# The first tile of w3 loaded, transposed and split in two halves, with the second tile's transposes behind the first products

## The chip, the cores and the metric

The kernel runs on one core of one Trainium2 chip. What counts is the time of one execution on the device in microseconds (us), and of several executions the median.

A core has engines that work side by side and meet at semaphores: TensorE (PE; its weight loads are listed apart as PEld), VectorE (DVE), ScalarE (ACT), GpSimd (POOL) and SyncE (SP), which here only issues DMAs. Each carries out its own list of instructions in order, so an instruction that waits holds up all behind it on its engine.

## The reference

Three layers stand in a row: attention in which a query sees only keys of its own hash bucket, a gated product of four matrices, and a mixture of four experts. The change lies in the weights of the second:

```python
def _moe_ref(x, w1, w2, w3, w_out) -> np.ndarray:
    a = x @ w1
    b = x @ w2
    h = a * b @ w3
    return (h @ w_out).astype(np.float32)
```

Here x has 1536 rows of 512 numbers, w1 and w2 are 512x1024, w3 is 1024x1024, w_out is 1024x512. In the attention there are 16 heads of 768 tokens with 64 numbers each; the experts have 512x1024 and 1024x512 weights. All is float32.

## The kernel before

**What happens first.** The kernel multiplies w3 by w_out once, at the very start, and uses the product (`wp_hi`, `wp_lo`) later. This takes eight steps (`it` = 0 to 7), one for each tile of 128 rows of w3. In each step TensorE transposes the tile in eight blocks of 128x128 (`transpose_w3`, through an identity matrix) into two PSUM banks; ScalarE copies the result as its high part to `w3T_hi` (`w3T_high`); VectorE subtracts that from PSUM for the low part `w3T_lo` (`w3T_low`); and TensorE multiplies (`multiply_wp`). float32 numbers are split in a high and a low part all over the kernel, and each product is made of three matmuls (`mult3`: high by high, low and high crossed both ways). So the step's product has eight blocks (`kt` = 0 to 7) of three matmuls of 512 columns, 24 in all, summed up in one bank.

**Buffers.** Tiles use two sets of buffers by turns (`par`): `w3_raw`, `w3T_hi`, `w3T_lo`, and the banks `ps01` and `ps23`. The trace calls `w3_raw` by the name `w_raw`, and in it all four PSUM tensors are `ps`.

**w_out.** It comes in four pieces of 512 KB (`stage` 0 to 3), each with the rows for two values of `kt`. ScalarE makes the high part of each (`wout_high(j)`), then VectorE the low one (`wout_low(j)`) and adds one to `wout_split`. In step 0 TensorE waits before each `kt` until `wout_split` is `kt // 2 + 1`: piece 0 for `kt` 0 and 1, piece 1 for 2 and 3, and so on.

**What sets the order.** All orders are written out by hand.
- SyncE issues the loads one after the other: tile 0 of w3, w_out pieces 0 and 1, tile 1, pieces 2 and 3, small constants, and then q, k and v of the first two heads. From then on it reloads `w3_raw` as soon as `w3T_mm` says that a tile is transposed.
- TensorE transposes tile 0 and tile 1 and only then starts the products of step 0. From step 1 on a part of the preparation of q and k (`first_prep`) and the transposes of the next tile stand between two steps.
- ScalarE: high part of tile 0, pieces 0 and 1, high part of tile 1, pieces 2 and 3.
- VectorE: low part of tile 0, pieces 0 and 1, low part of tile 1, pieces 2 and 3, then some small constants (`constants`), and then by turns `wp_low` and the low part of the next tile.
- GpSimd waits for the first q and k and splits them (`split_q`, `split_k`), each with a cast and a subtraction.

**Afterwards.** The attention runs over 8 pairs of heads, then come the gate products (a form of Strassen's method with seven products instead of eight), the product with `wp`, and the experts. There TensorE is nearly always busy. The change doesn't touch these parts.

Of the kernel before, what the change touches and what calls it, by code (L numbers as in the profile page):

```python
# [7 lines left out]
F32 = mybir.dt.float32  # L8
F32R = mybir.dt.float32r
BF16 = mybir.dt.bfloat16  # L10
ALU = mybir.AluOpType
# [9 lines left out]
def build_program(nc, q, k, v, proj, moe_w1, moe_w2, moe_w3, moe_w_out, probs, moe2_w1, moe2_w2,  # L21
                  codes, code_scalars, sum_rec, out):
    B, H, S, DH = q.shape
    D, F = moe_w1.shape
# [45 lines left out]
    with ExitStack() as ctx:  # L70
        def sem(name):
            return ctx.enter_context(nc.semaphore(name))
# [3 lines left out]
        def place(name, shape, dt, at=None):  # L76
            words = int(np.prod(shape[1:]))
            size = (words * (2 if dt == BF16 else 4) + 31) // 32 * 32
            offset = cursor[0] if at is None else at[0]
            if at is None:  # L80
                cursor[0] += size
            else:
                at[0] += size
            return nc.alloc_sbuf_tensor_at(name, shape, dt, offset=offset)
# [6 lines left out]
        w3_raw = [place(f"w3_raw{n}", [P, F], F32, w3_at) for n in range(2)]  # L91
        w3T_hi = [place(f"w3T_hi{n}", [P, FK, P], F32R, w3_at) for n in range(2)]
        w3T_lo = [place(f"w3T_lo{n}", [P, FK, P], F32R, w3_at) for n in range(2)]
# [132 lines left out]
        ps_w3T = [ps01, ps23]  # L226
# [6 lines left out]
        w3_loaded = [sem(f"w3_loaded{n}") for n in range(2)]  # L233
# [4 lines left out]
        e_loaded = [sem(f"e_loaded{n}") for n in range(SLOTS)]  # L238
        v2_loaded = [sem(f"v2_loaded{n}") for n in range(PIECES)]
        stored = sem("stored")  # L240
        zeros_set, ident_ready = sem("zeros_set"), sem("ident_ready")
        proj_hi_ready, proj_ready, code_ready = sem("proj_hi_ready"), sem("proj_ready"), sem("code_ready")
        gate_step, pool_held = sem("gate_step"), sem("pool_held")
        piece_hi, wout_split = sem("piece_hi"), sem("wout_split")
        w3T_mm, w3T_hi_done, w3T_lo_done = sem("w3T_mm"), sem("w3T_hi_done"), sem("w3T_lo_done")
# [24 lines left out]
        w3_tiles = moe_w3.rearrange("(i p) n -> i p n", p=P)  # L270
# [14 lines left out]
        def mult3(out_ps, lhs_hi, lhs_lo, rhs_hi, rhs_lo, start, stop, onto=False):  # L285

            nc.tensor.matmul(out_ps, lhs_hi, rhs_hi, start=start, stop=False, skip_group_check=onto)  # L287
            nc.tensor.matmul(out_ps, lhs_hi, rhs_lo, start=False, stop=False, skip_group_check=onto)  # L288
            return nc.tensor.matmul(out_ps, lhs_lo, rhs_hi, start=False, stop=stop, skip_group_check=onto)  # L289
# [4 lines left out]
        def _(sp):  # L294
# [77 lines left out]
                    ft = FT_ORDER[PIECES * h + p]  # L372
                    sp.dma_start(v2_raw[p][:, :], moe2_w2[e, ft * P:(ft + 1) * P, :]).then_inc(v2_loaded[p], 16)

            sp.dma_start(w3_raw[0][:, :], w3_tiles[0]).then_inc(w3_loaded[0], 16)
            for j in range(4):
                load_piece(j, tall(moe_w_out)[j])
                if j == 1:
# [285 lines left out]

        @block.scalar
        def _(act):
            def w3T_high(it, par, first):
                act.wait_ge(w3T_mm, it + 1)
                if not first:
                    act.wait_ge(wp_mm, it - 1)  # L670
                nc.scalar.copy(w3T_hi[par][:, :, :], ps_w3T[par][:, :, :]).then_inc(w3T_hi_done, 1)
# [5 lines left out]
            def wout_high(j):  # L677

                act.wait_ge(stage_loaded[j], 16)
                nc.scalar.copy(wout_hi[:, j * PIECE:(j + 1) * PIECE], stage[j][:, :]).then_inc(piece_hi, 1)  # L680
# [83 lines left out]
                    exp(1, 2)  # L764


            w3T_high(0, 0, True)
            wout_high(0)
            wout_high(1)
            w3T_high(1, 1, True)  # L770
            wout_high(2)
            wout_high(3)
# [5 lines left out]
            for it in range(1, FK):  # L778
                first_copy(2 * it - 2)
                wp_high(it - 1, (it - 1) % 2)  # L780
                first_copy(2 * it - 1)
                if it < FK - 1:
                    w3T_high(it + 1, (it + 1) % 2, False)
# [168 lines left out]
        @block.vector  # L952
        def _(dve):

            def w3T_low(it, par):
                dve.wait_ge(w3T_hi_done, it + 1)
                nc.vector.tensor_tensor(w3T_lo[par][:, :, :].rearrange("p (a c) n -> p a (c n)", a=2),
                                        ps_w3T[par][:, :, :],
                                        w3T_hi[par][:, :, :].rearrange("p (a c) n -> p a (c n)", a=2).bitcast(F32),
                                        ALU.subtract).then_inc(w3T_lo_done, 1)  # L960
# [7 lines left out]
            def wout_low(j):  # L968
                cols = slice(j * PIECE, (j + 1) * PIECE)
                dve.wait_ge(piece_hi, j + 1)  # L970
                nc.vector.tensor_tensor(wout_lo[:, cols], stage[j][:, :], wout_hi[:, cols].bitcast(F32),
                                        ALU.subtract).then_inc(wout_split, 1)
# [119 lines left out]
                    prep_code(n // GROUPS, n % GROUPS)  # L1092


            w3T_low(0, 0)
            wout_low(0)
            wout_low(1)
            w3T_low(1, 1)
            wout_low(2)
            wout_low(3)  # L1100
            constants()
            for it in range(1, FK):
                first_code(2 * it - 2)
                wp_low(it - 1, (it - 1) % 2)
                first_code(2 * it - 1)
                if it < FK - 1:
                    w3T_low(it + 1, (it + 1) % 2)
# [192 lines left out]
        def _(pe):  # L1300
# [1 line left out]


            def transpose_w3(it, par, first):
                pe.wait_ge(w3_loaded[par], 8 * it - 8 * par + 16)
                if not first:
                    pe.wait_ge(w3T_lo_done, it - 1)
                for kt in range(FK):
                    last = nc.tensor.transpose(ps_w3T[par][:, kt // 4, (kt % 4) * P:(kt % 4 + 1) * P],  # L1309
                                               w3_raw[par][:, kt * P:(kt + 1) * P], ident[:, :])  # L1310
                last.then_inc(w3T_mm, 1)

            def multiply_wp(it, par, first):
                pe.wait_ge(w3T_lo_done, it + 1)
                if not first:
                    pe.wait_ge(wp_lo_done, it - 1)
                for kt in range(FK):
                    if it == 0:
                        pe.wait_ge(wout_split, kt // 2 + 1)
                    if it == FK - 1 and kt in (2, 5):  # L1320

                        scores(kt // 3, 0, 0, kt // 3, kt == 2)
                    cols = slice(kt * D, (kt + 1) * D)
                    last = mult3(ps_wp[par], w3T_hi[par][:, kt, :], w3T_lo[par][:, kt, :],
                                 wout_hi[:, cols], wout_lo[:, cols], kt == 0, kt == FK - 1)
                last.then_inc(wp_mm, 1)
# [37 lines left out]
            def scores(g, i, s, t, first):  # L1364

                if t == 0:
                    pe.wait_ge(stacks_moved[s], 64 * (i + 1))
                if not first:
                    pe.wait_ge(score_scaled, g)
                for hf in range(2):  # L1370
                    half = slice(hf * HALF, (hf + 1) * HALF)
                    nc.tensor.matmul(ps_score[:, hf, 0:HALF], q_main[s][:, t * P:(t + 1) * P], k_main[s][:, half],  # L1372
                                     start=True, stop=False)
                    last = nc.tensor.matmul(ps_score[:, hf, 0:HALF], q_cross[s][:, t * P:(t + 1) * P],  # L1374
                                            k_cross[s][:, half], start=False, stop=True)
                last.then_inc(score_mm, 1)
# [82 lines left out]


            transpose_w3(0, 0, True)
            transpose_w3(1, 1, True)
            multiply_wp(0, 0, True)
            for it in range(1, FK):
                first_prep(2 * it - 2)
                if it < FK - 1:
                    transpose_w3(it + 1, (it + 1) % 2, False)
                first_prep(2 * it - 1)
                if it == FK - 1:
                    pe.wait_ge(w3T_lo_done, FK)  # L1470
                multiply_wp(it, it % 2, it == 1)
# [160 lines left out]
```

## Time and profile before

| what | value |
|---|---|
| median of 3 runs | 1017.78 us (1017.48 to 1018.08) |
| the profiled execution | 1016.71 us |
| its span, first to last instruction | 1014.8 us |
| TensorE busy | 991.9 us (98%) |
| VectorE busy | 638.2 us (63%) |
| ScalarE busy | 464.1 us (46%) |
| GpSimd busy | 402.9 us (40%) |
| TensorE busy in the first 30 us | 23.57 us |

The profile stems from one execution; its times are counted from the start of its span. The end of a matmul is modelled, so where matmuls follow each other closely their starts say more than their durations. The chain of waits is followed back from the last instruction and lists for each step what released it, or the instruction before it on its engine.

### The profile page before, as it was taken

What the parts mean: (1) busy time and instruction counts of PE and PEld (TensorE: products, weight loads), DVE (VectorE), ACT (ScalarE), POOL (GpSimd) and SP (SyncE); (2) the same over time, 40 slices, a digit from 0 to 9 for tenths busy, and PEclk for the clock granted to TensorE, in tenths of its full rate; (3) what the DMA queues carried; (4) which work ended last, traced back from release to release, by engine and by line L of the source; (5) the groups of instructions that cost most, each with busy time, mean ns of one, the idle gap of its engine ahead of it and who ended that gap; (6) DMA issues with size and microseconds to landing.
All of it is one profiled execution on the core that took longest, in us unless ns stands there. A gap on an engine that the chain in (4) does not pass through costs nothing.

```text
span 1014.8 us, 15947 instructions
## 1 busy us (share of the span) xinstructions
PE 991.9 (98%) x5520; PEld 922.2 (91%) x5520; DVE 638.2 (63%) x965; ACT 464.1 (46%) x871; POOL 402.9 (40%) x412
## 2 busy tenths in 40 slices
PE   7989999999998999999999999999999999999998
PEld 6879999999988999999998898989989899898997
DVE  5348889888997899198955354463544535345342
ACT  4238888878776554354543150331404215042230
POOL 4021333284533995295446051340603416034130
PEclk9999999999999999999999999999999999999999
DMA  6323333333233121010120110201102011010102
GB/s 239 94 70 95 94 102 97 113 94 93 86 87 91 52 78 43 7 57 10 34 63 21 42 42 1 63 21 43 42 1 62 21 41 41 1 61 21 41 12 112
DMA packets 56813, 60.58 MB, mean 60 GB/s; under 512 B 5600, under 2 KB 44736, under 8 KB 56768
## 3 DMA queue, kind: packets, MB, share of 16 engines
q1 hardware_dynamic: 56768, 60.00, 19.5%
q8 instruction: 26, 0.43, 0.2%
q14 instruction: 19, 0.16, 0.0%
HBM read 44.20 MB, written 3.19 MB: 47 GB/s over the span
## 4 chain that ended last, share of the span: by engine, by line
PE 89%; DVE 5%; issue 3%; ACT 2%; DMA 1%; SPq 0%; DVEq 0%; ACTq 0%
PE ps L287 23%; PE ps L288 23%; PE ps L289 23%; PE ps L1388 5%; PE ps L1401 3%; PE ps L1372 3%; PE ps L1403 3%; PE ps L1374 3%; PE ps L1345 1%; PE ps L1350 1%; DVE expo L989 1%; DVE w_lo L1023 1%; DVE hid_lo L1147 1%; ACT expo L691 1%; PE ps L1309 1%
## 5 line engine op out<-in xcount | busy, mean ns | idle before, releaser
L603 POOL TENSOR_TENSOR v_sum<-kept,kept 128x384 f32<-128x384 f32 x48 | 52.5, 1095 | 293.1 <-ACT kept L802 293.1
L1279 DVE SCALAR_TENSOR_TENSOR acc<-ps,gate,acc 128x512 f32<-128x512 f32 x96 | 72.0, 750 | 136.4 <-PE ps L289 136.4
L802 ACT COPY kept<-ps 128x384 f32<-128x384 f32 x144 | 64.1, 480 | 200.0 <-PE ps L289 199.4
L289 PE MATMUL ps<-v_hi,hid_lo 128*128 128x512 f32 x384 | 149.6, 390 | 0.0
L288 PE MATMUL ps<-v_lo,hid_hi 128*128 128x512 f32 x384 | 149.5, 389 | 0.0
L287 PE MATMUL ps<-v_hi,hid_hi 128*128 128x512 f32 x384 | 149.4, 389 | 0.0
L989 DVE TENSOR_SCALAR_CACHE_REDUCE expo<-ps 128x768 f32<-128x768 f32 x96 | 91.7, 955 | 24.7 <-PE ps L1374 24.7
L691 ACT ACTIVATE expo<-expo,neg_max 128x768 f32<-128x768 f32 x96 | 90.2, 940 | 8.3 <-DVE expo L989 6.7
L1266 DVE SCALAR_TENSOR_TENSOR hid_lo<-c,hid_hi 128x384 fp32r<-128x384 f32 x96 | 63.1, 669 | 46.2 <-ACT hid_hi L923 19.1
L1007 DVE TENSOR_TENSOR pT_lo<-ps,pT_hi 128x768 fp32r<-128x768 f32 x96 | 90.4, 947 | 1.5 <-ACT pT_hi L699 1.3
L289 PEld LDWEIGHTS ps<-v_hi,hid_lo 128*128 128x128 f32 x384 | 72.1, 188 | 15.0
L288 PEld LDWEIGHTS ps<-v_lo,hid_hi 128*128 128x128 f32 x384 | 72.1, 188 | 14.8
L287 PEld LDWEIGHTS ps<-v_hi,hid_hi 128*128 128x128 f32 x384 | 72.1, 188 | 14.8
L1128 DVE TENSOR_TENSOR u_sum<-ps,kept 128x384 f32<-128x384 f32 x48 | 26.6, 555 | 92.6 <-PE ps L289 90.7
L699 ACT CAST pT_hi<-ps 128x768 fp32r<-128x768 f32 x96 | 76.6, 799 | 14.8 <-PE ps L1388 14.4
L287 PE MATMUL ps<-xc_hi,w_hi 128*128 128x384 f32 x224 | 75.9, 339 | 1.4 <-ACT kept L802 1.4
L1388 PE MATMUL ps<-ident,expo 128*128 128x128 f32 x576 | 75.8, 273 | 0.6 <-DVE pT_lo L1007 0.6
L288 PE MATMUL ps<-xc_lo,e_hi 128*128 128x384 f32 x224 | 75.7, 338 | 0.0
L289 PE MATMUL ps<-xc_hi,e_lo 128*128 128x384 f32 x224 | 75.7, 338 | 0.0
L289 PE MATMUL ps<-xc_hi,w_lo 128*128 128x384 f32 x224 | 75.7, 338 | 0.0
L288 PE MATMUL ps<-xc_lo,w_hi 128*128 128x384 f32 x224 | 75.7, 338 | 0.0
L287 PE MATMUL ps<-xc_hi,e_hi 128*128 128x384 f32 x224 | 75.7, 338 | 0.0
(158 smaller groups left out, 2513.5 us busy)
## 6 DMA issues: line engine op xcount, KB each, us to landing
w_raw<-in_moe_w SPq DMA_DIRECT2D x64, 128.0 KB, 2.4
e_raw<-in_moe_w SPq DMA_DIRECT2D x64, 128.0 KB, 2.2
v_raw<-in_moe_w SPq DMA_DIRECT2D x32, 256.0 KB, 3.2
w_raw<-in_moe_w SPq DMA_DIRECT2D x8, 512.0 KB, 4.1
raw_q<-in_q SPq DMA_DIRECT2D x16, 192.0 KB, 2.8
raw_k<-in_k SPq DMA_DIRECT2D x16, 192.0 KB, 2.8
raw_v<-in_v SPq DMA_DIRECT2D x16, 192.0 KB, 2.7
q_main<-q_cross SPq DMA_DIRECT2D x16, 192.0 KB, 2.7
```

Of the source, the lines that this page charges most:

```text
L287: nc.tensor.matmul(out_ps, lhs_hi, rhs_hi, start=start, stop=False, skip_group_check=onto)
L288: nc.tensor.matmul(out_ps, lhs_hi, rhs_lo, start=False, stop=False, skip_group_check=onto)
L289: return nc.tensor.matmul(out_ps, lhs_lo, rhs_hi, start=False, stop=stop, skip_group_check=onto)
L603: nc.gpsimd.tensor_tensor(v_sum[:, :], kept[s][1][:, :], kept[s][2][:, :], ALU.add).then_inc(v_done, 1)
L691: nc.scalar.activation(expo[slot][:, :], expo[slot][:, :], ACT.Exp, scale=-1.0, bias=neg_max[:, slot:slot + 1], accum_out=row_sum[s][:, t: ...
L699: nc.scalar.copy(dst, ps_pT[t % 2][:, :, 0:HALF].rearrange("p a (c n) -> p a c n", n=P))\
L802: nc.scalar.copy(kept[s][n][:, :], ps[4 * s + n][:, 0:HALF]).then_inc(kept_done, 1)
L989: nc.vector.tensor_scalar(expo[slot][:, :].rearrange("p (a n) -> p a n", a=2), ps_score[:, :, 0:HALF], -SCALE, None, ALU.mult, ALU.min, ac ...
L1007: nc.vector.tensor_tensor(pT_lo[half][:, :, cols].rearrange("p (a c) n -> p a c n", a=2), ps_pT[t % 2][:, :, 0:HALF].rearrange("p a (c n) ...
L1266: nc.vector.scalar_tensor_tensor(hid_lo[:, tile, cols], src, 0.0, hid_hi[:, tile, cols].bitcast(F32), ALU.max, ALU.subtract).then_inc(hid_ ...
L1279: nc.vector.scalar_tensor_tensor(acc[:, t, :], ps[4 * ((h + t // 4) % 2) + t % 4], gate_f[:, bass.ds(t * E + e, 1)], acc[:, t, :], ALU.mul ...
L1388: last = nc.tensor.transpose(ps_pT[t % 2][:, kt // HT, (kt % HT) * P:(kt % HT + 1) * P], expo[slot][:, kt * P:(kt + 1) * P], ident[:, :])
```

## The change

Tile 0 of w3 is loaded with two DMAs, 512 columns each, the first of which has a semaphore of its own (`w3_first`). TensorE transposes blocks 0 to 3 after the first, and blocks 4 to 7 after the second. ScalarE and VectorE each handle the two halves with an instruction of their own, with semaphores for the first half (`w3T_first_mm`, `w3T_first_hi`, `w3T_first_lo`). The products of `kt` = 0 wait for the low part of the first half, and those of `kt` = 4 for that of the second. Tile 1's transposes are called in `multiply_wp(0, ...)` ahead of `kt` = 2. All later tiles are handled as before.

```diff
@@ block.sync
-            sp.dma_start(w3_raw[0][:, :], w3_tiles[0]).then_inc(w3_loaded[0], 16)
+            sp.dma_start(w3_raw[0][:, 0:F // 2], w3_tiles[0][:, 0:F // 2]).then_inc(w3_first, 16)
+            sp.dma_start(w3_raw[0][:, F // 2:F], w3_tiles[0][:, F // 2:F]).then_inc(w3_loaded[0], 16)
@@ block.scalar
+            def first_w3T_high():
+                act.wait_ge(w3T_first_mm, 1)
+                nc.scalar.copy(w3T_hi[0][:, 0:4, :].rearrange("p c n -> p (c n)"), ps_w3T[0][:, 0, :])\
+                    .then_inc(w3T_first_hi, 1)
+                act.wait_ge(w3T_mm, 1)
+                nc.scalar.copy(w3T_hi[0][:, 4:8, :].rearrange("p c n -> p (c n)"), ps_w3T[0][:, 1, :])\
+                    .then_inc(w3T_hi_done, 1)
...
-            w3T_high(0, 0, True)
+            first_w3T_high()
             wout_high(0)
             wout_high(1)
             w3T_high(1, 1, True)
@@ block.vector
+            def first_w3T_low():
+                for half, ready, done in ((0, w3T_first_hi, w3T_first_lo), (1, w3T_hi_done, w3T_lo_done)):
+                    tiles = slice(4 * half, 4 * half + 4)
+                    dve.wait_ge(ready, 1)
+                    nc.vector.tensor_tensor(w3T_lo[0][:, tiles, :].rearrange("p c n -> p (c n)"), ps_w3T[0][:, half, :],
+                                            w3T_hi[0][:, tiles, :].rearrange("p c n -> p (c n)").bitcast(F32),
+                                            ALU.subtract).then_inc(done, 1)
...
-            w3T_low(0, 0)
+            first_w3T_low()
@@ block.tensor
             def transpose_w3(it, par, first):
-                pe.wait_ge(w3_loaded[par], 8 * it - 8 * par + 16)
+                if first and it == 0:
+                    pe.wait_ge(w3_first, 16)
+                else:
+                    pe.wait_ge(w3_loaded[par], 8 * it - 8 * par + 16)
...
                 for kt in range(FK):
+                    if first and it == 0 and kt == 4:
+                        last.then_inc(w3T_first_mm, 1)
+                        pe.wait_ge(w3_loaded[par], 16)
...
             def multiply_wp(it, par, first):
-                pe.wait_ge(w3T_lo_done, it + 1)
+                if it:
+                    pe.wait_ge(w3T_lo_done, it + 1)
...
                     if it == 0:
+                        if kt == 2:
+                            transpose_w3(1, 1, True)
+                        if kt in (0, 4):
+                            pe.wait_ge(w3T_lo_done if kt else w3T_first_lo, 1)
                         pe.wait_ge(wout_split, kt // 2 + 1)
...
             transpose_w3(0, 0, True)
-            transpose_w3(1, 1, True)
             multiply_wp(0, 0, True)
```

The row of instructions on TensorE at the very start, before; `w_raw_51` and `w_raw_52` are the buffers of tile 0 and tile 1, `w3T_hi_53` and `w3T_lo_55` the two parts of tile 0:

```order
L1309 MATMUL ps<-ident,w_raw_51 128x128 [waits w3_loaded0,ident_ready]
L1309 MATMUL ps<-ident,w_raw_51 128x128 x7
L1309 MATMUL ps<-ident,w_raw_52 128x128 [waits w3_loaded1]
L1309 MATMUL ps<-ident,w_raw_52 128x128 x7
L287 MATMUL ps<-wout_hi,w3T_hi_53 128x512 [waits wout_split,w3T_lo_done]
L288 MATMUL ps<-wout_lo,w3T_hi_53 128x512
L289 MATMUL ps<-wout_hi,w3T_lo_55 128x512
L287 MATMUL ps<-wout_hi,w3T_hi_53 128x512 [waits wout_split]
L288 MATMUL ps<-wout_lo,w3T_hi_53 128x512
L289 MATMUL ps<-wout_hi,w3T_lo_55 128x512
```

and the same place after the change:

```order
L1335 MATMUL ps<-ident,w_raw_51 128x128 [waits w3_first,ident_ready]
L1335 MATMUL ps<-ident,w_raw_51 128x128 x3
L1335 MATMUL ps<-ident,w_raw_51 128x128 [waits w3_loaded0]
L1335 MATMUL ps<-ident,w_raw_51 128x128 x3
L290 MATMUL ps<-wout_hi,w3T_hi_53 128x512 [waits wout_split,w3T_first_lo]
L291 MATMUL ps<-wout_lo,w3T_hi_53 128x512
L292 MATMUL ps<-wout_hi,w3T_lo_55 128x512
L290 MATMUL ps<-wout_hi,w3T_hi_53 128x512 [waits wout_split]
L291 MATMUL ps<-wout_lo,w3T_hi_53 128x512
L292 MATMUL ps<-wout_hi,w3T_lo_55 128x512
L1335 MATMUL ps<-ident,w_raw_52 128x128 [waits w3_loaded1]
L1335 MATMUL ps<-ident,w_raw_52 128x128 x7
```

Tile 1's eight transposes have moved behind six matmuls of step 0, and tile 0's have been parted in four and four.

On ScalarE at the same place, before; `stage_72` to `stage_75` are the w_out pieces 0 to 3, and `w3T_hi_54` is tile 1's high part:

```order
L671 CAST w3T_hi_53<-ps 128x1024 [waits w3T_mm]
L680 CAST wout_hi<-stage_72 128x1024 [waits stage_loaded0]
L680 CAST wout_hi<-stage_73 128x1024 [waits stage_loaded1]
L671 CAST w3T_hi_54<-ps 128x1024 [waits w3T_mm]
L680 CAST wout_hi<-stage_74 128x1024 [waits stage_loaded2]
L680 CAST wout_hi<-stage_75 128x1024 [waits stage_loaded3]
```

and after:

```order
L673 CAST w3T_hi_53<-ps 128x512 [waits w3T_first_mm]
L676 CAST w3T_hi_53<-ps 128x512 [waits w3T_mm]
L692 CAST wout_hi<-stage_72 128x1024 [waits stage_loaded0]
L692 CAST wout_hi<-stage_73 128x1024 [waits stage_loaded1]
L683 CAST w3T_hi_54<-ps 128x1024 [waits w3T_mm]
L692 CAST wout_hi<-stage_74 128x1024 [waits stage_loaded2]
L692 CAST wout_hi<-stage_75 128x1024 [waits stage_loaded3]
```

The first cast has become two; the place of tile 1's cast between pieces 1 and 2 is the same. VectorE's list has changed in the same way.

## Rows read from the trace of the kernel before

**Rows 1.** The page, busy time of an engine with its share of the span

```profile
PE 991.9 (98%) x5520; PEld 922.2 (91%) x5520; DVE 638.2 (63%) x965; ACT 464.1 (46%) x871; POOL 402.9 (40%) x412
```

**Rows 2.** Waits of TensorE, whole span: us in total, times, longest

```profile
PE ps L1309 <- DMA w_raw<-in_moe_w: 6.4, 2, 4.2
PE ps L1372 <- DVE expo L989: 2.1, 2, 1.1
```

**Rows 3.** Timeline of TensorE: start, duration in us, instruction, count, idle before

```profile
4.23 1.94 PE L1309 MATMUL ps<-ident,w_raw 128*128 128x128 f32 x8 [4.23 <-DMA w_raw<-in_moe_w]
8.37 1.97 PE L1309 MATMUL ps<-ident,w_raw 128*128 128x128 f32 x8 [2.20 <-DMA w_raw<-in_moe_w]
9.99 0.78 PE L287 MATMUL ps<-wout_hi,w3T_hi 128*128 128x512 f32 x1
...
12.62 0.40 PE L287 MATMUL ps<-wout_hi,w3T_hi 128*128 128x512 f32 x1
...
17.09 1.04 PE L1309 MATMUL ps<-ident,w_raw 128*128 128x128 f32 x8
```

**Rows 4.** Chain of waits, 7 to 20 us: start, duration, what

```profile
2.17 6.15 DMA w_raw<-in_moe_w
...
16.70 0.23 PE ps L289
```

**Rows 5.** Windows: length, busy PE, PEld, DVE, ACT, POOL, granted clock, DMA share, GB/s

```profile
10.00:12.00 2.00, 2.00 (x7) 1.61 (x6) 1.32 (x2) 1.63 (x2) 0.00 (x0) 1.00 1.12 345
```

**Rows 6.** Timeline of ScalarE

```profile
7.11 1.05 ACT L680 CAST wout_hi<-stage 128x1024 fp32r<-128x1024 f32 x1
...
10.37 1.01 ACT L671 CAST w3T_hi<-ps 128x1024 fp32r<-128x1024 f32 x1 [1.26 <-PE ps L1309]
11.28 2.00 ACT L680 CAST wout_hi<-stage 128x1024 fp32r<-128x1024 f32 x2
...
17.67 0.60 ACT L675 CAST wp_hi<-ps 128x512 fp32r<-128x512 f32 x1
```

**Rows 7.** Timeline of VectorE

```profile
8.39 2.35 DVE L971 TENSOR_TENSOR wout_lo<-stage,wout_hi 128x1024 fp32r<-128x1024 f32 x2
...
12.56 2.66 DVE L971 TENSOR_TENSOR wout_lo<-stage,wout_hi 128x1024 fp32r<-128x1024 f32 x2
...
25.29 0.69 DVE L964 TENSOR_TENSOR wp_lo<-ps,wp_hi 128x512 fp32r<-128x512 f32 x1 [2.72 <-ACT wp_hi L675]
```

**Rows 8.** Timeline of SyncE's DMA issues: start, duration, tile, count

```profile
0.75 0.39 SPq L375 DMA_DIRECT2D w_raw<-in_moe_w  x1
1.20 0.93 SPq L297 DMA_DIRECT2D stage<-in_moe_w_out  x2
...
2.68 1.03 SPq L297 DMA_DIRECT2D stage<-in_moe_w_out  x2
```

**Rows 9.** Issue to landing, us: w3 tile 0, w_out piece 0, w_out piece 3

```profile
w_raw<-in_moe_w SPq DMA_DIRECT2D x1, 512.0 KB, 3.3
...
stage<-in_moe_w_out SPq DMA_DIRECT2D x1, 512.0 KB, 4.2
...
stage<-in_moe_w_out SPq DMA_DIRECT2D x1, 512.0 KB, 7.8
```

**Rows 10.** Timeline of TensorE's weight loads, at kt = 6

```profile
15.27 0.19 PEld L287 LDWEIGHTS ps<-wout_hi,w3T_hi 128*128 128x128 f32 x1 [0.17 <-DVE wout_lo L971]
```

**Rows 11.** The page, DMA issues: count, KB each, median us to landing

```profile
w_raw<-in_moe_w SPq DMA_DIRECT2D x64, 128.0 KB, 2.4
...
v_raw<-in_moe_w SPq DMA_DIRECT2D x32, 256.0 KB, 3.2
```

**Rows 12.** Timeline of GpSimd

```profile
12.84 1.30 POOL L471 CAST q_parts<-raw_q 128x384 fp32r<-128x384 f32 x1 [10.44 <-DMA raw_k<-in_k]
...
17.65 0.52 POOL L471 CAST q_parts<-raw_q 128x384 fp32r<-128x384 f32 x1
18.25 1.01 POOL L473 TENSOR_TENSOR q_parts<-raw_q,q_parts 128x384 fp32r<-128x384 f32 x1
```

More of the change, by code:

```diff
@@ L240, in build_program @@
         stored = sem("stored")
+        w3_first, w3T_first_mm, w3T_first_hi, w3T_first_lo = (
+            sem(n) for n in ("w3_first", "w3T_first_mm", "w3T_first_hi", "w3T_first_lo"))
         zeros_set, ident_ready = sem("zeros_set"), sem("ident_ready")
```

## The prediction

> **What bounds the kernel now.** I read the page's share of busy time first: TensorE is busy for 98% of the span [rows 1]. There is almost no room except where it waits, so a change at the start is worth what it moves TensorE's later work. The list of waits puts 6.4 us down to two waits for tiles of w3, 4.2 us until the first lands and 2.20 us ahead of the second tile's transposes [rows 2, 3].
>
> Next I read the chain of waits for 7 to 20 us [rows 4]: landing of the second w3 tile, its eight transposes, then the 24 products of tile 0, until 16.93 us. The first six take 2.63 us (9.99 to 12.62 [rows 3]), the last stand 0.23 us apart [rows 4]: the spacing falls from 0.43 or so to 0.23 us at about 12.5 us. 512 columns in 0.43 us are 1.2 GHz and in 0.23 us 2.4 GHz; the granted clock column says 1.00 in this stretch too [rows 5], so here I go by spacing. TensorE had worked without a break since 8.37 us, 4.1 us, when the clock rose.
>
> That chain hides a second one, nearly as late, and it decides this case. ScalarE and VectorE have one order each: tile 0's split, w_out pieces 0 and 1, **tile 1's split**, w_out pieces 2 and 3. In the timelines, ScalarE starts tile 1's high part at 10.37, behind the end of tile 1's transposes (8.37 + 1.97 = 10.34 [rows 3]), and then pieces 2 and 3 from 11.28 [rows 6]; VectorE finishes piece 3 at 12.56 + 2.66 = 15.22 us [rows 7]. Yet piece 3, the later, had landed at about 3.2 + 7.8 = 11.0 us [rows 8, 9]. At kt = 6 the weight loads already wait 0.17 us for piece 3 [rows 10]. So pieces 2 and 3 hang on the end of tile 1's transposes, and tile 0's products hang on pieces 2 and 3 with no slack.
>
> **The change, part by part.** All times are of the profiled execution (1016.71 us, span 1014.8; the median of the runs is 1017.78, 1.07 above).
>
> *Load in halves.* One DMA issue more; issues stand 0.45 us apart (0.75 to 1.20) [rows 8], so all behind it leaves 0.45 us later. The transfer engines are full meanwhile (share 1.12 [rows 5]), so the same bytes arrive at about the same time; I allow 0 to 0.45 us on each landing. Half a tile is 256 KB. Nearest rows: 128 KB in 2.4 us, 256 KB in 3.2 among three others of its kind [rows 11], and the whole 512 KB tile in 3.3 [rows 9]. So the first half lands 2.4 to 3.3 us after 0.75; I take 2.7, or 3.45. The second half is there with the last byte, 4.05 to 4.5; I take 4.2.
>
> *Transposes in halves.* Eight cost 1.62 us from the first to the following product (8.37 to 9.99), 0.20 each [rows 3]. First four from 3.5 to 4.3, second four to 5.15, with 0.35 us until the last result, as now (10.34 - 9.99): 5.5 instead of 6.17. Gain 0.7.
>
> *Splits in halves.* ScalarE's 128x512 cast costs 0.60 against 1.01 us for the whole tile [rows 6]; a following instruction starts some 0.1 before the end (10.37 + 1.01 against 11.28). The first half lies in the wait for the second, so piece 0 starts at 5.5 + 0.55 = 6.05 instead of 7.11. It has landed: 1.20 + 4.2 = 5.4 [rows 8, 9], at worst 5.85. Its cast takes 1.05, then VectorE's part 1.2 (two in 2.35) [rows 6, 7]: 7.15 to 8.35. VectorE's own halves (0.69 each by its 128x512 subtraction [rows 7]) end at 6.8 and are hidden. The first product starts at 8.4 instead of 9.99: **1.6 us earlier**. Piece 1 follows 1.2 later, at 9.6, before kt = 2 asks for it.
>
> *Tile 1's transposes behind the first products.* Six products now take 9.99 to 12.62, 2.63 us [rows 3]; from 8.4 they end at 11.0. Tile 1 landed at 2.17 + 6.15 = 8.32 [rows 4], so that wait is gone, and the old idle time is filled. The eight transposes then start at 11.0. All at the low clock they give their result 1.97 us later, 13.0; all at the high clock 1.04 later [rows 3], 12.05. The unbroken run again starts at 8.4, so I take the clock to rise at 12.5 as before: 12.7. That is **2.35 us later** than 10.34 (bounds 1.7 to 2.7).
>
> What is queued behind this wait: on ScalarE tile 1's high part, pieces 2 and 3, on VectorE their low parts and the constants; TensorE's kt = 4 to 7 wait for the pieces. All move by 2.35: piece 2 from 13.7 to 16.1, piece 3 from 15.2 to 17.6.
>
> *VectorE against GpSimd.* GpSimd's 384-element cast took 1.30 us beside VectorE's piece 2; later the cast took 0.52 and the subtraction behind it 1.01 [rows 12]. Two of VectorE's pieces together took 2.35, pieces 2 and 3 took 2.66, 0.3 more [rows 7]: it waited for the cast. GpSimd starts at 12.84, when its inputs land. VectorE now comes to pieces 2 and 3 only at 14.9, so GpSimd gets through q's cast and subtraction alone, and then subtractions of 1.01 us stand where a cast of 0.5 stood. Bounds: -0.3 (they never meet) to +1.2 (two meetings with a subtraction); I take +0.6, one subtraction instead of one cast. The Trainium skill (SBUF — State Buffer, section "SBUF: two separate sides") says that such a pair of instructions takes the shared port as an exclusive lock for the whole instruction. By that rule the later engine waits for the full rest of the other's instruction, which would make the term up to +0.7; the stretched cast fits it.
>
> *TensorE after that.* kt = 2 and 3 run from 12.65 to 14.0 (six at 0.23). Then a **new wait of 2.1 us** for piece 2 (16.1), six products to 17.5, and a wait for piece 3 at 17.6 + 0.6 = 18.2. Now it comes at 15.22, and what follows it is the same. Shift: 2.35 + 0.6 = 2.95, rounded to **+3.0 us**. The 1.6 us of the earlier start are spent in the new wait.
>
> *Later.* TensorE works almost without a gap from there [rows 1], and a later wait such as the one for scaled scores, 2.1 us in two [rows 2], is for VectorE work which TensorE feeds itself, so it moves along. VectorE's constants and tile 2's low part are queued behind piece 3 and move by 3.0 too; VectorE then stands idle for 2.72 us until 25.29 [rows 7], which moves likewise, so nobody waits for them. SyncE's reload of the second buffer waits for tile 1's transposes, 10.3 to 12.7; a 512 KB load takes 3.3 us alone [rows 9] and its use comes a whole tile's products later. No cost.
>
> The Trainium skill (TensorE: Matmul & The Clock Gate, "Part 4: PE-mode transpose") says that the full clock doesn't engage for transposes. The trace shows otherwise: eight took 1.94 us at 4.23 and 1.04 us at 17.09 [rows 3]. By the page they would end at 13.0 here and the sum would be +3.3.
>
> **The rivals.** *The clock is late or falls back.* The engine now stands for 2.1 us at 14.0, soon after the rise. For it: standing idle 2.2 us at 6.2, it worked at the low clock afterwards; against: it had not reached the high one before. Price: transposes 0.3 later and 12 products at 0.43 instead of 0.23 (2.4 us, some of it beside VectorE's piece 3): +3.6 to +5.5, middle 1022.3.
>
> *The clock rises earlier and GpSimd costs nothing.* If the earlier start of the products brings the rise forward to 11 us, the transposes end at 12.05 (+1.7), and without another meeting the shift is +1.4 to +2.0: 1019.5. For it: the rise now comes 2.5 us after the first product, which would be 10.9.
>
> *Not slower.* The 1.6 us gained stay, because tile 1's transposes end by 10.34 in spite of their new place, so that pieces 2 and 3 come no later. This decides at one point: a result of those transposes at 10.34 or before. It takes the high clock from about 5 us on: products 8.4 to 9.8 or some 0.3 sooner, transposes 1.04 more. Shift 0 to -0.8, 1017.4. No row shows the high clock so early.
>
> *The shift is absorbed.* TensorE's 2.1 us of waiting for the first scaled scores [rows 2] shrink to nothing, and +3.0 becomes +0.9 or less: 1018.7 down to 1017.8. Against: VectorE works there on what TensorE sends.
>
> **How the numbers follow.** Forecast (+2.2 to +3.6, at +3.0): 0.57. Clock late: 0.15. Clock early: 0.17. Absorbed: 0.07. Not slower: 0.04. Predicted: 1017.78 + 3.0 = 1020.8. The range 1019.0 to 1022.7 takes in the forecast, the early clock and most of the late clock, and leaves out about 0.18. A measurement of this kernel tells about 0.2% from no change, 2.04 us. Slower by over that: 0.57 + 0.15, or 0.72; within it: 0.17 + 0.07 and most of the last case, 0.26; faster by over that: 0.02.
>
> **What would show it.** First product near 8.4; tile 1's transposes from about 11.0 to 12.7, ScalarE's cast of it right behind; a wait of about 2 us of kt = 4 for VectorE's w_out piece; piece 3 near 18.2, tile 0's products ending near 19.9; the same distances from there to the end. I am wrong if kt = 4 doesn't wait, if spacing is 0.43 us beyond 14 us, or if the first tile's end has moved and the span has not.

## The result and the profile after

| | before | changed |
|---|---|---|
| median of 6 runs | 1017.93 us | 1022.06 us |
| lowest to highest | 1017.48 to 1019.01 | 1021.21 to 1024.66 |
| the profiled execution | 1016.71 us | 1024.66 us |
| its span | 1014.8 us | 1023.0 us |

The changed kernel is slower: ratio 1.0043, 95% interval 1.003 to 1.0056, or +4.1 us on the medians. The profiled execution is the slowest of its six, and that of before lay below all six of its own, so the 7.95 us between these two overstate the loss. They still show where it arises.

TensorE's waits over the whole span, us in total, times, longest (they answer [rows 2]):

```profile
PE ps L290 <- DVE wout_lo L991: 7.6, 2, 4.8
...
PE ps L1335 <- DMA w_raw<-in_moe_w: 3.5, 1, 3.5
PE ps L1403 <- DVE expo L1009: 2.1, 2, 1.1
```

The wait for the second tile of w3 is gone. In its place TensorE waits for VectorE's parts of w_out, 4.8 and 2.8 us. The later wait for scaled scores is exactly what it was.

The start on TensorE: start, duration, count, idle before (to set beside [rows 3]):

```profile
3.53 1.94 PE L1335 MATMUL ps<-ident,w_raw 128*128 128x128 f32 x8 [3.53 <-DMA w_raw<-in_moe_w]
...
10.28 0.77 PE L290 MATMUL ps<-wout_hi,w3T_hi 128*128 128x512 f32 x1 [4.80 <-DVE wout_lo L991]
...
12.97 1.91 PE L1335 MATMUL ps<-ident,w_raw 128*128 128x128 f32 x8
...
19.12 0.77 PE L290 MATMUL ps<-wout_hi,w3T_hi 128*128 128x512 f32 x1 [2.80 <-DVE wout_lo L991]
```

ScalarE's, VectorE's and GpSimd's timelines of the same stretch (for [rows 6, 7, 12]):

```profile
7.83 1.04 ACT L692 CAST wout_hi<-stage 128x1024 fp32r<-128x1024 f32 x1 [1.74 <-DMA stage<-in_moe_w_out]
...
14.92 1.02 ACT L683 CAST w3T_hi<-ps 128x1024 fp32r<-128x1024 f32 x1 [4.71 <-PE ps L1335]
```

```profile
17.11 3.30 DVE L991 TENSOR_TENSOR wout_lo<-stage,wout_hi 128x1024 fp32r<-128x1024 f32 x2
```

```profile
16.90 0.99 POOL L484 TENSOR_TENSOR k_parts<-raw_k,k_parts 128x384 fp32r<-128x384 f32 x1
17.84 1.50 POOL L475 CAST q_parts<-raw_q 128x384 fp32r<-128x384 f32 x1
```

Three things stand out.

1. The halves work as such: the tile's transposes start at 3.53 instead of 4.23. But ScalarE then stands 1.74 us for **w_out piece 0, which lands only at 7.8 us** (1.67 + 6.1), not at 5.4. The first product starts at 10.28, later than before.
2. Tile 1's transposes give their result at 14.90, ScalarE is right behind with 14.92, pieces 2 and 3 follow, and `kt` = 4 waits 2.80 us for piece 2. VectorE needs 3.30 us for the two pieces (1.86 and 1.52, the second starting before the first has ended), where it needed 2.66 before (1.22 and 1.52). The first runs into GpSimd's subtraction, which ends at 17.89.
3. After this wait TensorE works at half its clock. The windows show it; columns as in [rows 5]:

```profile
12.00:16.00 4.00, 4.00 (x17) 3.35 (x16) 0.03 (x1) 1.08 (x2) 1.14 (x2) 1.00 1.04 385
16.00:20.00 4.00, 1.20 (x4) 0.81 (x3) 4.00 (x3) 1.83 (x2) 3.84 (x5) 0.79 0.48 171
20.00:24.00 4.00, 4.00 (x11) 3.03 (x11) 3.93 (x12) 0.00 (x0) 3.84 (x5) 0.50 0.00 0
```

TensorE stands from 16.32 to 19.12 us, and the granted clock falls within that wait: in windows of half a microsecond it is 1.00 up to 18.0, 0.81 from 18.0 to 18.5 and 0.50 from 18.5 on. From 20 to 24 us it is 0.50, the 1.2 GHz level; in the chain of waits the last products of tile 0 stand 0.43 us apart:

```profile
23.73 0.43 PE ps L291
24.16 0.43 PE ps L292
24.58 0.64 PE ps L1376 x3
```

So tile 0 ends at 24.58 instead of 16.93. Afterwards the whole program is only moved. The wait for the one-hot codes and the first for scaled scores stand at 61.91 and 70.94 before:

```profile
61.91 0.34 PE L1354 MATMUL ps<-bits,code 128*128 128x384 bf16 x1 [0.84 <-DVE onehot L983]
...
70.94 0.44 PE L1372 MATMUL ps<-k_main,q_main 128*128 128x384 f32 x1 [1.06 <-DVE expo L989]
```

and 8.0 us later after, equally long:

```profile
69.91 0.34 PE L1385 MATMUL ps<-bits,code 128*128 128x384 bf16 x1 [0.84 <-DVE onehot L1003]
...
78.93 0.45 PE L1403 MATMUL ps<-k_main,q_main 128*128 128x384 f32 x1 [1.06 <-DVE expo L1009]
```

In this execution the steps of the loss are: the result of tile 1's transposes at 14.90 instead of 10.34, +4.56; piece 3 (17.11 + 3.30 = 20.41 instead of 15.22), +0.63 more; from there to the end of tile 0 4.17 instead of 1.71 us, +2.46, because the 12 products of `kt` = 4 to 7 stand 0.43 instead of 0.23 us apart, so that those of `kt` = 6 start only at 21.82, long after piece 3; a last 0.4 for the transposes behind, some of them at the low clock. That is the 8.0.

### The profile page after: what moved, and what is told of

Its sections match the earlier page's. It is cut to its first block, busy times and chain, and to the rows that moved or that the text cites. A ratio compares the mean times of both kernels' runs of the same rounds, so it can differ in the third digit from the quotient of the medians.

```text
span 1023.0 us, 15951 instructions
## 1 busy us (share of the span) xinstructions
PE 995.2 (97%) x5520; PEld 924.4 (90%) x5520; DVE 638.3 (62%) x966; ACT 464.4 (45%) x872; POOL 403.0 (39%) x412
## 4 chain that ended last, share of the span: by engine, by line
PE 88%; DVE 5%; issue 3%; ACT 3%; DMA 1%; DVEq 0%; SPq 0%; ACTq 0%
PE ps L290 23%; PE ps L291 23%; PE ps L292 23%; PE ps L1419 5%; PE ps L1432 3%; PE ps L1403 3%; PE ps L1434 3%; PE ps L1405 3%; PE ps L1376 1%; PE ps L1381 1%; DVE expo L1009 1%; DVE w_lo L1043 1%; DVE hid_lo L1167 1%; ACT expo L703 1%; PE ps L1335 1%
```

## The experiments

Each kernel was run beside the kernel before on the same chip; the times of before were 1017.66, 1017.75 and 1017.87 us in the three groups of four. "Clock 1.0" is the mean granted clock of a whole execution; a stretch at half clock shows as 0.996 to 0.998. Where nothing else is said, a kernel's executions lay at 0.999 or 1.0.

### The changed kernel again

No edit.

> The changed kernel once more, to see what repeats. Its profiled execution of before this run was 1024.66 us with piece 0 of w_out landing at 7.8 us (5.4 in the kernel before) and TensorE at the 1.2 GHz spacing again after a wait of 2.8 us. Theory A (the wait for w_out piece 2 behind tile 1's split is the cost, the fall of the clock comes with it): +3 to +4 us to the kernel before; executions in which the clock doesn't fall near +3, those in which it falls near +5. Theory B (the late landing of w_out is the cost, brought by the two half loads): piece 0 lands near 7.8 again.

1021.42 us, ratio 1.0038 (1.0024 to 1.0051). Piece 0 landed at 7.5 us, late again, and the clock fell again in the wait: products from 18.90 to 21.60 stand 0.43 us apart.

```profile
18.90 0.77 PE L290 MATMUL ps<-wout_hi,w3T_hi 128*128 128x512 f32 x1 [2.73 <-DVE wout_lo L991]
19.47 0.63 PE L291 MATMUL ps<-wout_lo,w3T_hi 128*128 128x512 f32 x1
...
21.60 0.49 PE L290 MATMUL ps<-wout_hi,w3T_hi 128*128 128x512 f32 x1
21.93 0.40 PE L291 MATMUL ps<-wout_lo,w3T_hi 128*128 128x512 f32 x1
```

Of the eleven executions of this kernel in both measurements, six had a clock of 0.996 to 0.998 (median 1022.99 us) and five had 1.0 (median 1021.21); one of the six, at 1021.45, lay below the slowest of the five, at 1021.83. Both theories seemed to hold in part, so they had to be parted.

### Halves alone

```diff
             transpose_w3(0, 0, True)
+            transpose_w3(1, 1, True)
             multiply_wp(0, 0, True)
...
-                        if kt == 2:
-                            transpose_w3(1, 1, True)
```

> Halves as in the change, but tile 1's transposes back ahead of the first products. Theory A: the result of tile 1's transposes is back at 10.3 to 10.8 us, w_out piece 3 at 15.2 to 15.7, and the time is the kernel before's within 0 to +0.6 us. Theory B (the two loads delay w_out by about 2 us): +1.5 to +2.5 us.

1018.9 us, ratio 1.001 (1.0001 to 1.0019): +1.2 us, between the two forecasts and barely clear of no change. Its profiled execution, the slowest of eleven, shows the loads late by 2.5 to 2.9 us: piece 0 at 8.3, tile 1 at 2.64 + 8.2, so that its transposes start at 10.88 (8.37 in [rows 3]). DMA issues, issue to landing (for [rows 9]): the two halves, piece 0, tile 1.

```profile
w_raw<-in_moe_w SPq DMA_DIRECT2D x1, 256.0 KB, 2.6
...
w_raw<-in_moe_w SPq DMA_DIRECT2D x1, 256.0 KB, 3.0
...
stage<-in_moe_w_out SPq DMA_DIRECT2D x1, 512.0 KB, 6.6
...
w_raw<-in_moe_w SPq DMA_DIRECT2D x1, 512.0 KB, 8.2
```

The halves themselves come early (3.35 and 4.2). What comes behind is late, although the issues are only 0.46 us later.

### The moved transposes alone

```diff
                     if it == 0:
+                        if kt == 2:
+                            transpose_w3(1, 1, True)
                         pe.wait_ge(wout_split, kt // 2 + 1)
...
             transpose_w3(0, 0, True)
-            transpose_w3(1, 1, True)
             multiply_wp(0, 0, True)
```

> The kernel before with the one edit that tile 1's transposes stand ahead of kt = 2; no halves. Theory A: first product at 9.65, six products to 12.3, transposes' result at 13.6 to 14.3, w_out piece 3 at 19 to 20: +3.7 to +4.5 us, and up to +6.5 where the clock falls in the wait. Theory B: w_out lands as before, so the time is within +1 us.

1021.38 us, ratio 1.0041 (1.0027 to 1.0054), +3.7 us. First product at 9.85 us, high part of tile 1 at 14.02 instead of 10.37, VectorE 3.30 us for the two pieces, and the new wait:

```profile
9.85 0.77 PE L287 MATMUL ps<-wout_hi,w3T_hi 128*128 128x512 f32 x1 [3.59 <-DVE wout_lo L971]
...
18.12 0.50 PE L287 MATMUL ps<-wout_hi,w3T_hi 128*128 128x512 f32 x1 [2.75 <-DVE wout_lo L971]
```

**Theory A holds for the greater part**: this edit alone brings a loss as large as the whole change. Here the clock stayed up in the profiled execution, after a wait of the same length as the one of 2.73 us behind which it fell; in two of five executions it fell. The three in which it stayed up have a median of 1021.13 us: without any fall of the clock, moving the transposes costs this kernel +3.5 us.

### Pieces 2 and 3 ahead of tile 1's split

```diff
             wout_high(1)
-            w3T_high(1, 1, True)
             wout_high(2)
             wout_high(3)
+            w3T_high(1, 1, True)
```

and the same on VectorE, both in the changed kernel.

> The changed kernel with ScalarE and VectorE doing w_out pieces 2 and 3 ahead of tile 1's split. Theory A: kt = 4 doesn't wait any more, tile 0's products end at 16 to 17.3 us (16.93 in the kernel before), tile 1's split is done before step 1's products ask for it at about 18.4, and the time is the kernel before's within -1.0 to +0.5 us. Theory B: the late w_out stays, +1.5 to +2.5 us.

1018.72 us, ratio 1.0009 (1.0 to 1.0018), +1.1 us, at the edge of what can be told from no change. `kt` = 4 doesn't wait. The wait for pieces 2 and 3 is what the move costs; with this order it costs nothing, in spite of the same place of the transposes. What is left is the load: piece 0 landed at 8.1 us, first product at 10.56.

### The changed kernel with one load

```diff
-            sp.dma_start(w3_raw[0][:, 0:F // 2], w3_tiles[0][:, 0:F // 2]).then_inc(w3_first, 16)
-            sp.dma_start(w3_raw[0][:, F // 2:F], w3_tiles[0][:, F // 2:F]).then_inc(w3_loaded[0], 16)
+            sp.dma_start(w3_raw[0][:, :], w3_tiles[0]).then_inc(w3_loaded[0], 16)
```

Both groups of four transposes wait for it.

> The changed kernel with tile 0 loaded by one DMA again; its transposes, splits and order stay as changed. Four kernels with the two column halves showed the transfers slow between 3.5 and 5.5 us (80 to 270 GB/s in half a microsecond, 350 to 400 in the kernels with one load) and w_out piece 0 landing at 7.5 to 8.3 us. Theory C (the two half loads slow the loads behind them): no such dip, piece 0 at 5.5, first product near 9.0, and 0.5 to 1.5 us less than the changed kernel, that is +2.3 to +3.3 us to the kernel before. Theory D (a chance of those executions): dip and time as in the changed kernel.

1020.25 us, ratio 1.0033 (1.0022 to 1.0043), +2.5 us. Piece 0 at 6.0 us, first product at 9.17. Five of its eight executions had clock 1.0, with a median of 1020.07 us, +2.3; the three others lay at 1021.76 to 1023.59. The changed kernel at clock 1.0 lay at 1021.21, so the half loads cost 1.1 us. The moved transposes alone had cost +3.5 at clock 1.0, with the same single load. This kernel differs from that one only in the halved transposes and splits: its first product starts at 9.17 instead of 9.85 us and tile 1's cast at 13.03 instead of 14.02. So the halved work does give back about 1 us. The bytes moved tell the same; transfers from 3.5 to 4.5 us, of the kernel before, of the halves alone and of this one:

```profile
DMA packets 195, 0.37 MB, mean 375 GB/s; under 512 B 14, under 2 KB 14, under 8 KB 195
```

```profile
DMA packets 61, 0.11 MB, mean 111 GB/s; under 512 B 7, under 2 KB 7, under 8 KB 61
```

```profile
DMA packets 188, 0.37 MB, mean 373 GB/s; under 512 B 7, under 2 KB 7, under 8 KB 188
```

The five profiled executions with both column halves on SyncE's queue gave 111 to 268 GB/s here and piece 0 at 6.5 to 8.3 us; every one with the single load gave 344 or more and 5.4 to 6.0. Theory C stands.

### One load and pieces first

Both edits together.

> The changed kernel with one load of tile 0 and with w_out pieces 2 and 3 split ahead of tile 1. Theory A (the whole loss lies in the pieces behind tile 1's split and in the half loads): nothing waits for either, tile 0's products end at 16.0 to 17.0 us, and the time is the kernel before's within -0.8 to +0.3 us.

1017.35 us, ratio 0.9996 (0.9987 to 1.0005). The whole loss is gone with these two. There were eleven executions, all at clock 1.0. Nothing measurable is gained over the kernel before, though the first product starts 0.8 us earlier than in [rows 3]: TensorE idles 2.97 us ahead of it, where it idled 2.20 us ahead of tile 1's transposes, and these now lie between the products. The last product of tile 0 starts at 17.38 us.

```profile
9.17 0.77 PE L290 MATMUL ps<-wout_hi,w3T_hi 128*128 128x512 f32 x1 [2.97 <-DVE wout_lo L990]
...
17.38 0.39 PE L292 MATMUL ps<-wout_hi,w3T_lo 128*128 128x512 f32 x1
```

### The wait filled

```diff
+                        if kt == 4:
+                            for n in range(9):
+                                nc.tensor.matmul(ps6[:, 0, :], w3T_hi[0][:, 0, :], wout_hi[:, 0:D],
+                                                 start=True, stop=True)
                         if kt in (0, 4):
                             pe.wait_ge(w3T_lo_done if kt else w3T_first_lo, 1)
```

> The changed kernel with nine more matmuls of 512 columns between kt = 3 and kt = 4, into a PSUM bank that nobody reads at that time; they fill 2.1 us of the wait for w_out piece 2. Theory A1 (the clock falls because the engine stands in that wait): no stretch at the 1.2 GHz spacing behind 17 us, the executions lie closer together, and the median is 0.3 to 1.2 us below the changed kernel's in spite of the added work. Theory A2 (the clock plays no part in the median): the time is the changed kernel's or up to 1 us more.

1020.96 us, ratio 1.0034 (1.0021 to 1.0048), all five executions at clock 1.0 and within 1.2 us. The median lies 0.5 us below that of the changed kernel in its repetition, and 1.1 below its first measurement. The difference of the medians alone is within the intervals; what is clear is the clock, and the next run repeats it.

### One load, the wait filled

> The changed kernel with one load of tile 0 and with nine more matmuls in the wait of kt = 4. Without the half loads and without a fall of the clock only the order of the pieces behind tile 1's split is left. In the kernel with the single load and no filling, executions with granted clock 1.0 lay at 1020.1 us and those below at 1021.8 to 1023.6. Expected: every execution at granted clock 1.0, +2.0 to +2.8 us to the kernel before. If the clock isn't caused by the wait: some executions above 1021.5 us again.

1020.39 us, ratio 1.0026 (1.0015 to 1.0037), seven executions, all at clock 1.0. With the unfilled moves (the changed kernel, its repetition, the moved transposes alone and the one load) the clock fell in 11 of 24 executions; with filled waits in 0 of 22 (this run, the last and the next). **The clock falls because TensorE stands in the new wait.** Where it falls, it costs 1.5 to 2.0 us (medians of the executions with and without a fall, in the changed kernel, the moved transposes alone and the one load). What is left with one load and the clock up is +2.3 to +2.5 us: the later pieces, less what the halved transposes and splits give back.

### GpSimd held back

```diff
                 split_q(s, 0, s, True)
+                if s == 0:
+                    pool.wait_ge(wout_split, 4)
                 split_k(s, s)
```

in the kernel of the last run.

> The kernel of the run whole_filled, in which GpSimd waits between its split of the first q and the first k until VectorE has done w_out piece 3. It prices the meeting of VectorE and GpSimd. If VectorE's two pieces (3.3 us together in the other kernels with the moved transposes, 2.35 alone) are slowed by GpSimd: 2.4 us now, piece 3 0.9 us earlier, +1.2 to +1.9 us to the kernel before. If not: pieces and time as in whole_filled.

1020.08 us, ratio 1.0022 (1.0012 to 1.0031), 0.3 us less than without (the executions of either kernel spread over 1.3 to 1.4 us). VectorE's two pieces without the hold, and with it:

```profile
15.69 3.16 DVE L990 TENSOR_TENSOR wout_lo<-stage,wout_hi 128x1024 fp32r<-128x1024 f32 x2
```

```profile
16.11 2.35 DVE L992 TENSOR_TENSOR wout_lo<-stage,wout_hi 128x1024 fp32r<-128x1024 f32 x2
```

The 0.8 us are GpSimd's doing. But only a part reaches the end: with the hold, piece 3 is there at 18.46, while the six products of `kt` = 4 and 5 keep TensorE until 18.93. Set off from the cast of tile 1's high part (13.50 and 13.92 us in the two executions), `kt` = 6 starts 5.41 us later without and 5.01 with the hold: 0.4 us. The forecast of 0.9 had taken VectorE's gain for the kernel's.

### Two row halves in the kernel before

```diff
-            sp.dma_start(w3_raw[0][:, :], w3_tiles[0]).then_inc(w3_loaded[0], 16)
+            sp.dma_start(w3_raw[0][0:P // 2, :], w3_tiles[0][0:P // 2]).then_inc(w3_first, 16)
+            sp.dma_start(w3_raw[0][P // 2:P, :], w3_tiles[0][P // 2:P]).then_inc(w3_loaded[0], 16)
```

> The kernel before with tile 0 loaded by two DMAs of 64 rows by 1024 columns; all else as before, and the transposes wait for both. One more DMA issue, but rows of 4 KB as in the single load, where the column halves have 2 KB. If the number of issues slows the loads behind: a dip between 3.5 and 5.5 us and piece 0 past 7 us, +1 us as for the halves alone. If the 2 KB rows do it: no dip, piece 0 at 5.4 to 5.9, +0 to +0.5 us.

1018.45 us, ratio 1.0008 (0.9999 to 1.0017), +0.7: between the two forecasts, and not clear of no change. Rows of 4 KB don't bring the transfers back: 223 GB/s from 3.5 to 4.5 us and piece 0 at 2.01 + 4.8 = 6.8. But these DMAs also take 0.58 us to issue instead of 0.39, the tile itself was complete only at 5.6 us, and the transfer engines were busy all the while (share 1.00, where the column halves had 0.61 to 0.81). So this run doesn't settle what slows the column halves.

### The halves in two queues

```diff
@@ block.sync
-            sp.dma_start(w3_raw[0][:, 0:F // 2], w3_tiles[0][:, 0:F // 2]).then_inc(w3_first, 16)
@@ block.scalar
+            act.dma_start(w3_raw[0][:, 0:F // 2], w3_tiles[0][:, 0:F // 2]).then_inc(w3_first, 16)
```

in the kernel with pieces first, where both on one queue had cost 1.1 us.

> The changed kernel with w_out pieces 2 and 3 ahead of tile 1's split, in which the first column half of tile 0 is loaded from ScalarE's queue and the second from SyncE's, at the same time. With both on SyncE's queue this kernel took +1.1 us and its piece 0 landed at 8.1 us. If the half loads hurt because they stand in one queue with the loads behind: piece 0 lands at 5.4 to 6.0 and the time is -0.6 to +0.3 us. If rows of 2 KB hurt wherever they are issued: piece 0 past 6.5, +0.7 to +1.3 us.

1017.51 us, ratio 1.0 (0.9991 to 1.0009). Piece 0 landed at 1.20 + 4.3 = 5.5 us. Transfers from 3.5 to 4.5 us:

```profile
DMA packets 211, 0.39 MB, mean 387 GB/s; under 512 B 22, under 2 KB 22, under 8 KB 211
```

Halves with the same 2 KB rows do no harm when one comes from another queue. **The harm comes with both half loads standing ahead of the pieces in one queue.** With two queues the pieces also leave 0.46 us earlier (1.20 instead of 1.66), but piece 0 lands 2.6 us earlier. What in the queue runs dry is open: in the halves-alone run the transfer engines were even less busy there (share 0.73 from 3.5 to 4.5 us) than in the kernel before (0.99). The early half is lost in this variant: with both at once they land at 4.35 and 4.15, as late as the whole tile.

### The order of the pieces alone, in the kernel before

> The kernel before with only w_out pieces 2 and 3 split ahead of tile 1. The wait of 0.17 us at kt = 6 goes, and tile 1's split comes at 12 to 14.6 us, ahead of its first use at 18.4. Expected: -0.4 to 0.0 us. It tells whether the 0.4 us by which the changed kernel with one load and this order lay under the kernel before need the halves and the moved transposes at all.

1017.63 us, ratio 1.0 (0.9991 to 1.0009). The wait of 0.17 us in [rows 10] was worth nothing that can be measured, and none of the three kernels without a loss is faster than the kernel before.

## Why the prediction came out as it did

**Right**: the direction, the mechanism and its place. The forecast was that pieces 2 and 3 hang on tile 1's transposes in ScalarE's and VectorE's fixed order, and that moving these costs a new wait of about 2 us at `kt` = 4. The measured waits are 2.31 to 2.80 us; the moved transposes alone bring +3.7 us, and the other order of the pieces takes the loss away. That the later waits move along held as well: they have the same lengths, 8.0 us later. The first half landed at 3.35 us (3.45 forecast). The term for VectorE against GpSimd had the right size at VectorE: 3.30 us is 0.64 more than before, +0.6 was forecast. Its reason was half right. VectorE didn't meet a subtraction instead of a cast but a subtraction and a cast: its first piece starts at 17.11, when 0.78 us of GpSimd's subtraction are left, and takes 0.64 longer than alone (1.86 against 1.22); its second takes 1.52, just as long as in the kernel before, where it also met a cast. The exclusive lock of which the Trainium skill speaks (SBUF — State Buffer, "SBUF: two separate sides") fits that.

**The size**: +3.0 was forecast, +4.1 measured, inside the range of 1019.0 to 1022.7. Two steps came out too low and one too high, so the landing in the range is in part luck.

- *"The same bytes arrive at about the same time"* is the step that failed. It allowed 0 to 0.45 us for the landings and took nothing for the time. Piece 0 came 2.4 us late in the profiled execution, the first product at 10.28 instead of 8.4, and the half loads cost 0.7 to 1.5 us in four pairs of kernels: 1.2 (halves alone against before, which also differ in the halved transposes and splits), 1.1 (changed against one load, at clock 1.0), 0.7 (the two filled kernels), 1.5 (the two with pieces first). The row that I read, a share of 1.12, lies at 10 to 12 us, and the transfers run short at 3.5 to 5.5. But reading that stretch of the trace before would not have warned me: its share from 3.5 to 4.5 us was 0.99, with 375 GB/s. The mistake was to carry a rate of the old kernel over to a queue with one more DMA at its head; there the share was 0.61.
- *The clock.* I took it to rise at 12.5 us and to stay up, and gave its fall 0.15. It fell in 6 of 11 executions of the changed kernel, at 1.8 us each, so some 1 us on the average. The rival's middle lay 1.5 us over my forecast, and 1.5 to 2.0 is what a fall costs. That its time of 1022.3 also lies near the 1022.99 of those executions is in part chance, since they hold the 1.1 us of the half loads too. My argument against it, that TensorE had never been seen to fall from the high level, was the absence of a row, not a row.
- *The move itself*, forecast at +3.0 with the gain of the halves in it, was +2.3 to +2.5 at clock 1.0 with one load (+3.5 without the halved transposes and splits). So the earlier start isn't wholly "spent in the new wait", as the prediction says: with one load the first product starts 0.7 us earlier than with the moved transposes alone, all behind it comes earlier too, and the kernel is about 1 us faster. For the rest, one part is that the sum was set against an execution at the low end of its kind: it lay 1.1 us under the median. In the profiled execution of the kernel before with pieces first, tile 1 landed at 9.1 instead of 8.3 us; in the order of before TensorE waits for that, with the moved transposes it doesn't. How much each of these makes isn't measured. Another part is GpSimd: +0.6 was forecast for the kernel; held back, it gives the kernel 0.3 to 0.4, because TensorE's six products lie beside it.

Taken together: 2.3 for the move, 1.1 for the loads and about 1 for the clock make 4.4, against 4.1 and 3.8 measured. The intervals reach about 1 us to each side, so the parts are no finer than that.

"The clock rises earlier" assumed a rise 2.5 us after the first product. With one load it came some 2.8 us after it, and the eight transposes took 1.12 us; in the other profiled executions with moved transposes it took up to 5.7 us. So it is one case of several, and the forecast should have held a range here, not 12.5. "Absorbed" is refuted by the later waits, which kept their lengths, and "not slower" by the result of tile 1's transposes, at 14.90 and not at 10.34.

## What to carry to other kernels

Before moving work back on the engine that is the bottleneck, list what the helper engines do *behind* the consumer of that work; in a fixed order it all moves by as much. Don't carry a full DMA rate over to a kernel whose queue begins otherwise; a second load at the head of a queue can delay all behind it by more than its issue, and only a trace of the changed queue shows it. And price a new wait of the bottleneck engine twice, by its length and by the clock that may be lost with it.

## What the hardware showed unexpectedly

- Two 256 KB loads in place of one of 512 KB at the head of one queue lowered the transfers from 3.5 to 4.5 us to 111-268 GB/s, against 344-389 in the kernels with one load, and not when they were in two queues (387).
- TensorE fell from the 2.4 GHz level (products 0.23 us apart) to 1.2 GHz (0.43 us, granted clock 0.50) in a wait of 2.73 or 2.80 us that began 1.1 to 1.3 us after the first products 0.23 us apart; it stayed up through waits of 2.31 and 2.75 us that began some 2.1 to 2.3 us after the spacing had changed. Two cases of each are too few to say that this is the difference. Filling the wait with 2.1 us of matmuls kept it up in 22 of 22 executions.
- The granted clock column said 1.00 at the start of each program, where the same spacing of 0.43 us stood. In that stretch the spacing is the better witness.
